# Moving weight transforms, ring loads and one moment inside a hand-ordered mixer kernel

## The reference

```python
q_s = exp(q - max(q, -1)); q_s /= sum(q_s, -1) + 1e-9
k_s = exp(k - max(k, 2));  k_s /= sum(k_s, 2) + 1e-9
x = q_s @ (k_s^T @ v)                          # stage A, per head
u = x + (relu(x^T @ w_tok1) @ w_tok2)^T        # stage A, token mixing: 576 -> 256 -> 576
y = u + relu(u @ w_ch1) @ w_ch2                # stage B: 512 -> 1536 -> 512
n = (y - mean(y)) / sqrt(var(y) + 1e-6) * g_ln
out = y + relu(n @ w_ch1c) @ w_ch2c            # stage C: 512 -> 2048 -> 512
```

## Time and profile before

| | before |
|---|---|
| median of 3 executions | 1529.94 us (1529.3 to 1534.36) |
| the profiled execution's own time | 1523.87 us |
| its span | 1522.1 us |
| TensorE busy | 1474.3 us (97%) |
| VectorE busy | 1051.9 us (69%) |
| ScalarE busy | 686.6 us (45%) |
| GpSimd busy | 265.1 us (17%) |
| DMA | 407.26 MB, mean 268 GB/s |

### The profile page before, as it was taken

One profiled execution on the slowest core, in us unless ns is written; L12 is line 12 of the kernel. 1 busy time (PEld: TensorE's weight loads), 2 busy tenths in 40 slices (PEclk: granted clock), 3 DMA queues, 4 the chain that ended last, 5 costly groups with the idle time before them and its releaser, 6 DMA issues.

```text
span 1522.1 us, 19959 instructions
## 1 busy us (share of the span) xinstructions
PE 1474.3 (97%) x7656; PEld 1328.4 (87%) x7656; DVE 1051.9 (69%) x1187; ACT 686.6 (45%) x862; POOL 265.1 (17%) x280
## 2 busy tenths in 40 slices
PE   5999999999999999899999999999999999999998
PEld 5999998878888888788888888888888888889997
DVE  7989874684693693696885686578568756872276
ACT  5656564542543543544533543454245324532342
POOL 6455565562121221210000000000000000000000
PEclk9999999999999999999999999999999999999999
DMA  7787839899888989988777768766876777677766
GB/s 243 243 265 239 275 117 372 316 351 352 312 307 310 369 315 306 350 304 271 268 254 268 243 221 279 237 232 232 280 244 218 258 253 251 205 231 250 252 209 201
DMA packets 138718, 407.26 MB, mean 268 GB/s; under 512 B 13568, under 2 KB 35392, under 8 KB 138624
## 3 DMA queue, kind: packets, MB, share of 16 engines
q1 hardware_dynamic: 123024, 347.00, 67.9%
q0 software_dynamic: 15600, 58.99, 10.4%
HBM read 326.24 MB, written 79.69 MB: 267 GB/s over the span
## 4 chain that ended last, share of the span: by engine, by line
PE 78%; DMA 9%; DVE 8%; issue 2%; ACT 1%; POOL 1%; SPq 1%; DVEq 0%; ACTq 0%
PE ps L1425 25%; PE ps L1427 25%; PE ps L1426 25%; DMA w_ring<-w_scratch_B 5%; DMA w_scratch_B<-w_out 2%; DVE x_lo L1047 1%; PE ps L1449 1%; DMA w_scratch_C<-side_out 1%; PE ps L1540 1%; PE ps L1460 1%; DMA qt<-q 1%; DVE o_lo L1100 1%; DVE w_out L1094 1%; DVE o_lo L1288 1%; DVE k_max L954 1%
## 5 line engine op out<-in xcount | busy, mean ns | idle before, releaser
L1425 PE MATMUL ps<-x_hi,w_ring 128*128 128x462 f32 (+1 forms) x920 | 343.4, 373 | 12.4 <-DMA w_ring<-w_scratch_B 9.2
L1425 PE MATMUL ps<-o_hi,w_ring 128*128 128x462 f32 (+1 forms) x920 | 343.1, 373 | 5.0 <-DVE o_lo L1288 2.7
L1427 PE MATMUL ps<-x_hi,w_ring 128*128 128x462 f32 (+1 forms) x920 | 342.1, 372 | 0.0
L1427 PE MATMUL ps<-o_hi,w_ring 128*128 128x462 f32 (+1 forms) x920 | 341.5, 371 | 0.0
L1426 PE MATMUL ps<-o_lo,w_ring 128*128 128x462 f32 (+1 forms) x920 | 341.5, 371 | 0.0
L1426 PE MATMUL ps<-x_lo,w_ring 128*128 128x462 f32 (+1 forms) x896 | 332.9, 372 | 0.0
L890 ACT CAST o_hi<-h 128x924 fp32r<-128x924 f32 (+1 forms) x189 | 182.0, 963 | 234.4 <-PE ps L1427 223.4
L1288 DVE TENSOR_TENSOR o_lo<-h,o_hi 128x924 fp32r<-128x924 f32 (+1 forms) x189 | 212.5, 1126 | 62.6 <-ACT o_hi L890 62.6
L1425 PEld LDWEIGHTS ps<-x_hi,w_ring 128*128 128x128 f32 x920 | 173.1, 188 | 38.5 <-issue 11.9
L1425 PEld LDWEIGHTS ps<-o_hi,w_ring 128*128 128x128 f32 x920 | 173.1, 188 | 31.5 <-issue 10.4
L1427 PEld LDWEIGHTS ps<-o_hi,w_ring 128*128 128x128 f32 x920 | 173.0, 188 | 19.3
(11 more groups left out here) (172 smaller groups left out, 2132.3 us busy)
## 6 DMA issues: line engine op xcount, KB each, us to landing
w_ring<-w_scratch_C SPq DMA_DIRECT2D x280, 512.0 KB, 4.2
w_ring<-w_scratch_B SPq DMA_DIRECT2D x168, 512.0 KB, 5.0
w_scratch_C<-w_out POOLq DMA_DIRECT2D x13, 1792.0 KB, 12.2
w_scratch_B<-w_out POOLq DMA_DIRECT2D x12, 1792.0 KB, 13.0
kt<-kT SPq DMA_DIRECT2D x32, 288.0 KB, 6.4
u_scratch<-u_out SPq DMA_DIRECT2D x32, 288.0 KB, 3.0
qt<-q SPq DMA_DIRECT2D x32, 256.0 KB, 4.9
ke<-k SPq DMA_DIRECT2D x32, 256.0 KB, 5.0
```

The lines of the kernel that those rows point to most:

```text
L1425: mm(dst, a_hi, b_hi, start=start, stop=False, skip_group_check=onto)
L1427: return mm(dst, a_lo, b_hi, start=False, stop=stop, skip_group_check=onto)
```

## The change

Five edits, numbered here as the prediction does.

1. Unit 0: GpSimd's four additions go from step 7 to step 6, two ahead of `sub_q` and two behind it. ScalarE's cast goes from the middle of step 7 to the end of step 6. GpSimd's additions for the first B unit (`sum_unit(AHEAD)`) go behind the store of unit 0.
2. SyncE's first three ring loads go from behind the last side store to behind the first, with a wait for the end of plain unit 3.
3. The residual loads of supergroup 0 wait in addition for the end of plain unit 9.
4. The entries of `HI_AT`: (0, 8, 27) becomes (3, 10, 28) in supergroup 1, and (1, 6, 11, 27) becomes (1, 8, 15, 28) in supergroups 2 and 3.
5. Moment 1 of the first normalization goes from behind (1, 2) to behind (1, 3); variance, root and newton follow by one place.

```diff
@@ NORM_AT[0]
-         "moment 1": (1, 2), "variance": (1, 3), "root": (1, 3), "newton": (1, 4),
+         "moment 1": (1, 3), "variance": (1, 4), "root": (1, 4), "newton": (1, 5),
@@
-    HI_AT = ((0, 8, 27), (1, 6, 11, 27), (1, 6, 11, 27), (4,))
+    HI_AT = ((3, 10, 28), (1, 8, 15, 28), (1, 8, 15, 28), (4,))
@@ SyncE
             for i in range(SIDE):
                 if i + 1 < SIDE:
                     load_side(i + 1)
                 store_side(i)
-            for n in range(RW - 1):
-                load_entry(n)
+                if i == 0:
+                    sp.wait_ge(groups, unit_over(3))
+                    for n in range(RW - 1):
+                        load_entry(n)
+            sp.wait_ge(groups, unit_over(9))
             sp.wait_ge(side_stored, 16 * SIDE)
@@ GpSimd, step (sum_unit is cut into first_sums and last_sums, the same four additions)
                 if later:
+                    if i == NB - 2:
+                        first_sums(0)
                     sub_q(i + 1, ST)
+                    if i == NB - 2:
+                        last_sums(0)
                     lo_q(i + 1)
                     return
-                sum_unit(0)
-                sum_unit(AHEAD)
                 lo_unit(0, 0)
                 lo_unit(0, 1)
                 load_unit(AHEAD + 1)
                 store_unit(0)
+                sum_unit(AHEAD)
@@ ScalarE, step
-                if later == 0:
-                    hi_unit(0)
...
                 if later:
                     hi_q(i + 1, ST[3:])
+                if i == NB - 2:
+                    hi_unit(0)
```

More of the change, by code:

```diff
@@ L553, in sum_unit, with first_sums @@
             def sum_unit(n):
+                first_sums(n)
+                last_sums(n)
+            def first_sums(n):
                 x = w_op[:, SLOT[n], :, :]
@@ L558, in sum_unit, with last_sums @@
                 nc.gpsimd.tensor_tensor(x[:, 4, :], x[:, 0, :], x[:, 7, :], ALU.subtract).then_inc(wp_sum, 1)
+            def last_sums(n):
+                x = w_op[:, SLOT[n], :, :]
                 pool.wait_ge(wp_sum, 4 * n + 1)
```

## The result

The changed kernel is slower: 1535.16 us (median of 20 runs, 1530.34 to 1539.5) against 1529.65 us for the kernel before (20 runs, 1526.39 to 1534.36). The ratio is 1.0037, 95% interval 1.0027 to 1.0047, so 4.1 to 7.2 us more. The prediction was 1519, faster. The profiled execution of the changed kernel took 1530.46 us, its span 1528.7.

The account below looks back on a forecast made before the run. TensorE, busy 97% of the span, was taken as the bound, so only its waits could be won. 6.9 + 3.9 - 1.4 + 1.6 = 11.0 us off the median 1529.94 gave 1519; range 1514 to 1523, with rivals 1511 to 1526.

Parts of the forecast that it names:

- edits 1 to 3: Plain stage: 1.5 us kept of a 2.5 us lead, plus 5.4 from the wait at 333.10 and its clock: 6.9 won.
- edit 5: Moment of the first normalization: one more entry of work (2.5 us) covers TensorE's wait for `s_lo`, 1.6 us won.
- edit 4 with entry 15's price: Supergroups 1 to 3: 3.9 us won on ring waits, less 1.4 us for work put into the third calls.
- Edit 4, the ring waits: Stores every 7 entries no longer overlap: supergroup 2 gains 0.9 us, supergroup 3 2.5, supergroup 1 0.5; 3.9 in all.
- the waits of supergroups 2 and 3 near 3 us each: Sign that the forecast is right: ring waits there, 3.7 and 5.3 us before, fall to about 3 each.
- a TensorE that waits there gives the ring time to catch up: Third calls of supergroups 2 and 3: reason to take 1.4 us as entry 15's price, not 2.2.
- the price of entry 15: Third calls of supergroups 2 and 3: a cast and two subtractions cost 1.4 us together, bounds 0 and 3.4.
- Does that lead of 2.5 us last?: Plain stage: the lead lasts only if the units' chain moves too; 1.5 us kept, bounds 0 and 2.7.
- so nothing is late: Residual loads start behind plain unit 9, wanted behind unit 11: 20 us of room for 1.9 MB.
- no edit here shortens it: First ring load behind the plain stage takes 8.9 us; the prediction left that unchanged.
- the first stage gives it back: Rival, 0.12: ring loads push the side store, plain unit 7 starts no earlier, 6.9 us is lost: 1526.
- VectorE's next consumer two entries behind; bounds 1.0 and 1.6: First normalization: variance and root may come one entry later; the gain of 1.6 us has bounds 1.0 and 1.6.

Follow-up runs that it names:

- entry 15: Kernel before with the third C unit of supergroups 2 and 3 at entry 15 for 11: 1535.42 us, ratio 1.0054.
- the two on the norm's table: Kernel before with variance, root and newton one place later, moment in place: 1532.16 us; kernel before with only the moment one place later: 1526.82 us.
- all improvements together: Kernel before plus edits 1 to 3, side casts behind, later inputs, C units at 3, 10, 27 and twice 1, 7, 13, 27, later additions: 1520.20 us.
- the same with the moment later: All improvements together, with moment 1 one place later while variance, root and newton stay: 1520.28 us, ratio 0.9947 against the kernel before.

## Why the prediction was wrong

| term | predicted | part run alone |
|---|---|---|
| edits 1 to 3 | 6.9 won | 1.8 won (0.2 to 3.4) |
| edit 4 with entry 15's price | 2.5 won | 4.9 lost (3.1 to 6.6) |
| edit 5 | 1.6 won | 2.8 lost (1.2 to 4.4) |

**Edit 4, the ring waits.** Forecast were "the waits of supergroups 2 and 3 near 3 us each"; they are 3.4 and 1.9, a fall of 3.7 us for the 3.4 put down. That is in part luck. With the same spacing, where TensorE's waits in the third calls are shorter, the ring waits there are 8.3 and 7.1 us against 9.0 before. So a good part of the fall came as the prediction itself had it, "a TensorE that waits there gives the ring time to catch up", and what the spacing itself gives in these traces is 0.7 to 1.9 us at most. Supergroup 1, which was to keep its 1.4, went from 1.3 to 3.0.

**Edit 4, the price of entry 15** was the largest miss. The prediction saw that the unit's cast and two subtractions meet a VectorE nearly without slack, which is where the wait came, and put 0.7 each, bound 3.4 together. It counted what entry 15 puts on VectorE and ScalarE and left out what follows on GpSimd: the store, then four additions for the next unit beside VectorE's last operations. The Trainium skill (SBUF — State Buffer, "SBUF: two separate sides") has VectorE with two SBUF inputs and GpSimd exclude each other for a whole instruction; the trace agrees, 3.99 us for 2.14. I had used that rule in step 7 and not here. Second, the clock fell at the waits of 2.51 and 2.61, 0.43 x 4 = 1.7 us and 0.28 x 4 = 1.1 in the windows shown (the second begins before its fall and ends inside it). The two third calls cost 5.1 of waits (0.5 before) and 2.8 or more of clock, against 1.4. The prediction had counted this cost of the clock at the wait that went (333), and not at the waits it put in.

**Edits 1 to 3.** The step that failed is "Does that lead of 2.5 us last?", and the claim "so nothing is late" behind it. Up to the end of the plain stage the forecast was good: over at 348.67 (about 348 forecast), the store issued at 311 lands in 9.3 us. The 348.67 is a lucky one, though: in the five other traces with edits 1 to 3 and the side casts in their old place the stage is over at 350.69 to 353.58, against 354.95 to 358.94 with the old first stage. And a wait of 2.94 us at unit 7, which was to be absent, was there. But the argument looked for the lead's end only inside the stage. Behind it showed a first load of 8.9 us for a need of 7.5, and I noted that "no edit here shortens" it, without seeing that every edit lengthens it: the row says that transfers set the pace there, and then an earlier end is given back. Of the rivals, "the first stage gives it back" named the right term and the wrong place; that the edits pushed the side store is not shown, for its 14.3 us lie among the 13.0 to 15.0 of the six traces with the old first stage.

**One execution.** The case against that rival was that unit 7 had waited only 0.2 us. In the five other traces with the old first stage (edit 4, edit 5, entry 15 and the two on the norm's table) it waits 1.70, 2.38, 3.27, 4.00 and 1.81 us: the profiled execution of before, 6.1 us under the median, was the lucky one at just that place. I had seen the 6.1 and took it for an offset of the whole.

**Edit 5.** The step "VectorE's next consumer two entries behind; bounds 1.0 and 1.6" failed. The consumer that decides is ScalarE's cast `x_hi` at the far end of the chain, 0.12 us behind its operand before the change. A bound for a loss was missing.

**The baseline and the rest.** Edit 1's step 6 was hidden as forecast: neither the 0.7 at `u_out` nor the 1.8 at 237.6 came back, and no new wait stands there. Alone it measured 1.0002 (0.9986 to 1.0017), which is no gain, though one of up to 2.1 us is not excluded.

## What to carry to other kernels

A wait that goes in one stage is a gain only if the next stage can start early: look at how full the transfers are behind it, and ask what the first late load would do with a lead. When work moves, follow its whole train on every engine, the helper's next task included, and check where VectorE and GpSimd then meet (3.99 us for 2.14 here). A chain that ends as its consumer starts has no slack, whatever its first step waits for. A wait of 0.2 us read from one execution is no evidence of room. A wait that falls while another appears beside it may only have moved, so read it again in a run where the other is gone.

## What the runs showed of the hardware

- The clock. Waits of 3.31, 2.51, 1.95 and 2.61 us in the changed kernel each had a fall to the lower level (1.2 GHz) with them or just behind; one of 2.94 (297.14) and one of 2.12 (563.52) had none, nor had 2.52 and 2.02 in the kernel before. Length alone does not decide. In the run of entry 15 alone the fall at the wait of 3.25 us covered nearly the whole window of 7 us (0.51); with the waits there split into 1.03, 0.62 and 1.40 us (subtractions on GpSimd) the clock did not fall.
- One trace and its clock. Up to 710 us "all improvements together" and the same with the moment later run the same program, with the same median (1520.20 and 1520.28). The profiled execution of the one had falls at 47, 402 and 634 us and took 1523.89 us; that of the other had none there and took 1515.61.
- VectorE and GpSimd slow each other both ways: VectorE's 1.1 us operation took 2.57 beside GpSimd's subtractions, and GpSimd's addition of 0.74 took 2.81 beside a busy VectorE.
- A ring load of 512 KB took 4.3 us alone. Issued from 348.5 to 361 us it took 9.9 in the kernel before, 14.2 with edit 3 alone and 12.8 with edits 1 to 3; on top of these, 10.1 with the first C unit at entry 3, 6.9 with the inputs moved behind the ring loads, and 6.7 with both.
